# Loads of the values: window edges in two pieces, both batches in one request, values in fours split at partition 64

## The reference

```
# branch 1: positions averaged in fours (144 of them), full softmax attention, repeated 4 times
q_d = q.reshape(B, H, 144, 4, D).mean(axis=3)      # k_d, v_d likewise
out_up = np.repeat(softmax(q_d k_d^T / sqrt(D)) v_d, 4, axis=2)
# branch 2: every position attends to the positions less than 4 away
mask = np.abs(pos[:, None] - pos[None, :]) < 4
out_local = softmax(where(mask, q k^T / sqrt(D), -1e9)) v
x = (out_up + out_local) as 2304 tokens x 512
# layer 1: x / rms(x) * rms_g, then (silu(x w_gate) * (x w_val)) w_out, width 1536
# layer 2: relu(x w_in)^2 w_out, width 2048
```

## Time and profile before

| what | value |
|---|---|
| median of 3 runs | 960.91 us (960.46 to 963.03) |
| the profiled execution | 963.09 us |
| its span, first to last instruction | 961.3 us |
| mean granted TensorE clock | 0.978 |
| PE busy | 926.8 us, 96% |
| DVE, ACT, POOL busy | 648.3, 447.9, 588.7 us |
| DMA | 63.94 MB, mean 67 GB/s |

### The profile page before, as it was taken

The page is one execution under the profiler, slowest core; times in us unless marked ns, Lnnn a source line. Parts: engine busy times, 40 slices in busy tenths (PEclk is TensorE's granted clock), DMA queues, the critical chain, the costliest instruction groups (busy, mean ns, idle before and its releaser), DMA issues.

```text
span 961.3 us, 17765 instructions
## 1 busy us (share of the span) xinstructions
PE 926.8 (96%) x6056; PEld 837.6 (87%) x6056; DVE 648.3 (67%) x960; ACT 447.9 (47%) x1149; POOL 588.7 (61%) x627
## 2 busy tenths in 40 slices
PE   5879989999999999999999999999999999999998
PEld 5657768999999999999999998989898998989896
DVE  5859995678986668876455776667875456745353
ACT  3758785644455634455444464424342324333221
POOL 2458677778778867877766775555654445453520
PEclk9979878999999999999999999999999999999999
DMA  6566211321211111111111122121112101030101
GB/s 178 180 206 210 82 35 33 89 77 54 68 45 44 45 45 45 45 45 45 44 46 54 54 69 88 44 88 45 45 36 97 45 23 44 23 110 23 45 1 65
DMA packets 57961, 63.94 MB, mean 67 GB/s; under 512 B 5904, under 2 KB 50832, under 8 KB 57488
## 3 DMA queue, kind: packets, MB, share of 16 engines
q1 hardware_dynamic: 56288, 61.63, 20.8%
q10 hardware_dynamic: 1584, 1.18, 0.4%
HBM read 58.07 MB, written 4.72 MB: 65 GB/s over the span
## 4 chain that ended last, share of the span: by engine, by line
PE 77%; DVE 3%; issue 1%; ACT 1%; POOL 0%; DMA 0%; ACTq 0%; DVEq 0%
PE bank L1437 42%; PE bank L1492 20%; PE bank L1467 14%; DVE xs L1079 1%; ACT wst L698 0%; ACT xs L739 0%; DVE vt L1146 0%; DVE prod L1152 0%; PE bank L1447 0%; DVE wst L1086 0%; POOL wst L576 0%; DMA out_dram<-xT 0%; DVE gt L1146 0%; DVE wo L1191 0%; ACT xT L822 0%
## 5 line engine op out<-in xcount | busy, mean ns | idle before, releaser
L1437 PE MATMUL bank<-xs,wst 128*128 128x384 f32 x2520 | 505.1, 340 | 4.1 <-DVE vt L1146 2.4
L1437 PEld LDWEIGHTS bank<-xs,wst 128*128 128x128 f32 x2520 | 442.7, 189 | 28.6 <-issue 8.5
L576 POOL TENSOR_TENSOR wst<-wraw,wst 128x256 fp32r<-128x256 f32 x240 | 223.9, 952 | 143.0 <-ACT wst L698 141.7
L1492 PE MATMUL bank<-wo,gs 128*128 128x512 f32 x864 | 218.4, 393 | 1.4 <-ACT xT L822 0.8
L1467 PE MATMUL bank<-hb,wo 128*128 128x512 f32 x864 | 189.1, 336 | 1.3 <-DVE hb L1164 1.3
L1492 PEld LDWEIGHTS bank<-wo,gs 128*128 128x128 f32 x864 | 160.4, 188 | 29.8 <-DVE gs L1185 1.1
L1467 PEld LDWEIGHTS bank<-hb,wo 128*128 128x128 f32 x864 | 146.0, 188 | 9.9 <-issue 1.6
L1146 DVE TENSOR_TENSOR vt<-u,bank 128x384 f32<-128x384 f32 x120 | 66.2, 552 | 126.1 <-PE bank L1437 125.8
L698 ACT CAST wst<-wraw 128x256 fp32r<-128x256 f32 x360 | 123.1, 407 | 1.9 <-DMA wraw<-w_dram 1.2
L559 POOL TENSOR_TENSOR wraw<-wraw,stage 128x256 f32<-128x256 f32 x60 | 48.9, 815 | 96.5 <-DMA wraw<-w_dram 96.5
L785 ACT ACTIVATE sig<-gt 128x384 f32<-128x384 f32 x72 | 37.9, 526 | 124.8 <-DVE gt L1146 123.7
(11 more groups left out here) (110 smaller groups left out, 1054.5 us busy)
## 6 DMA issues: line engine op xcount, KB each, us to landing
wraw<-w_dram SPq DMA_DIRECT2D x180, 128.0 KB, 2.3
stage<-w_dram SPq DMA_DIRECT2D x60, 128.0 KB, 2.1
woraw<-w_dram SPq DMA_DIRECT2D x28, 256.0 KB, 3.0
vquad<-v_dram SPq DMA_DIRECT2D x16, 288.0 KB
out_dram<-xT SPq DMA_DIRECT2D x18, 256.0 KB, 2.9
vwin<-v_dram SPq DMA_DIRECT2D x56, 70.0 KB
kp<-k_dram SPq DMA_DIRECT2D x3, 1152.0 KB, 8.6
qs<-q_dram SPq DMA_DIRECT2D x3, 1152.0 KB, 11.0
```

Of the source, the lines that this page charges most:

```text
L576: nc.gpsimd.tensor_tensor(b[:, 1, :], w_source(w, p), b[:, 0, :].bitcast(fp32), ALU.subtract).then_inc(wlp_done, 1)
L1437: last = mm(XY[s % 2][:, 0:HC], wst[:, u % 2, p, pw, 128 * k:128 * k + 128], xs[:, p, px, k, :], start=(p not in CONTINUES and i == 0 and ...
L1492: last = mm(ACC[t][:, :], gs[:, v % 2, m, px, 128 * t:128 * t + 128], wo[:, 2 * j + m, pw, :], start=(j == 0 and n < 18 and i == 0), stop= ...
```

## The change

`load_v` now issues one request per unit for both batches of the group, with the batch as an inner dimension, where it issued two. For the first and the last unit, whose windows have 67 rows, it issues two such requests, of 64 and of 3 rows. That makes 11 requests per group where there were 18. `load_vquad` splits each of its four requests at partition 64, into 64 and 8 partitions. The waits count the new numbers of requests (`v_loads`, and 128 for 64 in `sum_values`). The same bytes go to the same places, in the same order on SyncE.

```diff
--- before.py
+++ after.py
@@ -389,6 +389,10 @@
         def head0(b):
             return NH * (b % 2)
 
+
+        def v_loads(u0, u1):
+            return u1 - u0 + (u0 == 0) + (u1 == NL)
+
         def down(g):
             i = g % NU - NL
             return i // 2, i % 2
@@ -405,21 +409,25 @@
         @block.sync
         def _(sp):
 
+
             def load_v(b, u0, u1, done):
                 for i in range(u0, u1):
                     t0, t1 = max(QB * i - HALO, 0), min(QB * i + QB + HALO, S)
-                    r0 = t0 - (QB * i - HALO)
-                    for x in range(2):
-                        src = v_d[batch0(b) + x][t0:t1, D * head0(b):D * head0(b) + GC]
-                        sp.dma_start(vwin[b % 2][r0:r0 + t1 - t0, x, i, :], src).then_inc(done, 16)
+                    r0 = QB * i - HALO
+                    for a, e in ((t0, t1),) if t1 - t0 == KW else ((t0, t0 + QB), (t0 + QB, t1)):
+                        src = v_d[batch0(b):batch0(b) + 2, a:e, D * head0(b):D * head0(b) + GC]
+                        sp.dma_start(vwin[b % 2][a - r0:e - r0, :, i, :],
+                                     src.rearrange("x r n -> r x n")).then_inc(done, 16)
+
 
             def load_vquad(b):
                 ready(sp, vd_done, 3 * b)
                 for x in range(2):
                     for kt in range(2):
                         v = v_d[batch0(b) + x][S // 2 * kt:S // 2 * kt + S // 2, D * head0(b):D * head0(b) + GC]
-                        sp.dma_start(vquad[:, kt, x, :, :],
-                                     v.rearrange("(p r) n -> p r n", r=FACTOR)).then_inc(vq_in, 16)
+                        fours = v.rearrange("(p r) n -> p r n", r=FACTOR)
+                        sp.dma_start(vquad[0:64, kt, x, :, :], fours[0:64]).then_inc(vq_in, 16)
+                        sp.dma_start(vquad[64:HK, kt, x, :, :], fours[64:HK]).then_inc(vq_in, 16)
 
             def rows_of(src, b, t0, t1):
                 return src[batch0(b):batch0(b) + 2, :, head0(b):head0(b) + NH, t0:t1].rearrange("b d h s -> (b d) h s")
@@ -980,7 +988,7 @@
             def sum_values(b, n):
 
                 if n == 0:
-                    dve.wait_ge(vq_in, 64 * (b + 1))
+                    dve.wait_ge(vq_in, 128 * (b + 1))
                     ready(dve, pv_done, NU * b)
                 else:
                     dve.wait_ge(vd_done, 3 * b + n)
@@ -1382,13 +1390,13 @@
                     pe.wait_ge(oe_done, g - 1)
                 if local(g):
                     if b == 0 and i == 0:
-                        pe.wait_ge(v_part[0], 32 * V_PARTS[0])
+                        pe.wait_ge(v_part[0], 16 * v_loads(0, V_PARTS[0]))
                     if b == 0 and i == V_PARTS[0]:
-                        pe.wait_ge(v_part[1], 32 * (V_PARTS[1] - V_PARTS[0]))
+                        pe.wait_ge(v_part[1], 16 * v_loads(V_PARTS[0], V_PARTS[1]))
                     if b == 0 and i == V_PARTS[1]:
-                        pe.wait_ge(v_in[b], 32 * (NL - V_PARTS[1]))
+                        pe.wait_ge(v_in[b], 16 * v_loads(V_PARTS[1], NL))
                     if b > 0 and i == 0:
-                        pe.wait_ge(v_in[b], 32 * NL)
+                        pe.wait_ge(v_in[b], 16 * v_loads(0, NL))
                     for x in range(2):
                         for a in range(NH):
                             c = QB * (2 * x + a // 2)
```

## The result

The changed kernel took 954.61 us as the median of 12 executions (947.97 to 961.93), the one before 960.94 (lowest 960.46). The ratio over all executions is 0.9921, interval 0.9892 to 0.9950, and that of the medians 0.9934: faster by 0.7 to 0.8%, where 1.6% was forecast, and just outside the range. But the profiled execution, the fastest of the twelve, took 947.97 us, 15.1 less than the profiled one before, and the forecast was 15.2. The median and the trace tell different stories because the executions of this kernel fall into two clusters. Of 24 timed (12 here, 12 in the run `again`) 9 lie from 947.9 to 953.1, 2 at 956 to 957, and 13 from 957.9 to 961.9. The mean clock goes with them: 0.983 to 0.989 in the first cluster, 0.971 to 0.978 in the last.

The account below looks back on a forecast made before the run. Bound: attention-stage loads on SyncE's queue, late because 67-row loads run on one engine. Gains 5.6 + 9.6 = 15.2 us took the profiled 963.09 to 947.9, median 945.7; forecast's own range 939 to 951, overall 939 to 954.

Parts of the forecast that it names:

- The mechanism of the gain: Attention stage: splitting 67-row loads takes away 11.4 us of one-engine work per group, so loads land before they are wanted.
- both waits: VectorE's 4.2 us wait for K's third piece and matmul's 7.6 us wait for group 1's windows, both forecast gone.
- the clock: Half-clock stretches from 100.3 and 131 us: may change, up to 4.7 us gained or 5 lost; taken as nothing.
- 5.6, 9.6 and 0: Forecast gains in us: up to Q of group 1, at group 1's windows, and from the late clock.
- Issue costs: SyncE's unblocked window requests per group: 7.2 us before, 5.6 after (4.1 to 9.2); group 1's issued by about 25 us.
- When the loads land: Attention stage: bytes set landing times at 278 GB/s after 5.6 us; K's third piece at 12.8 us, no wait left.
- Rival 3: Requests over two batches move slowly; at 70 GB/s group 1's windows land 19 us late: about 980 us; chance 0.03.
- Windows of group 1: They land at 32.7 us, wanted at 41.1; the 7.6 us matmul wait goes, gaining 9.6 us (7.6 to 10.4).
- one more stretch of 10 us: Rival 4: one more 10 us half-clock stretch in the part where matmul is full, 950.7 us; chance 0.05.
- Q of group 1 next late: Before unit 13: Q of group 1 lands at 28.1 us, wanted at 31.4; at 214 GB/s it lands at 34.8.
- rival 1: Loading group 1's K and Q replaces the wait: 949.2 us at 214 GB/s, 959.8 at 165, middle 954; chance 0.12.

Follow-up runs that it names:

- again: The changed kernel once more, unaltered; median 958.18 us (947.91 to 961.09), 12 executions, ratio to before 0.994.
- windows_only: The changed kernel with the `load_vquad` requests (the fours) left whole: merged windows with split edges; median 950.98 us, ratio to before 0.9887.
- edges_only: The kernel before with only the 67-row requests split into 64 and 3 rows, one request per batch, fours whole; median 949.85 us, ratio 0.9875.
- again_c: One more execution of the unaltered changed kernel, with its trace; 960.02 us.
- again_b: One more execution of the unaltered changed kernel, with its trace; 950.83 us.
- edges_gap: Kernel with only the 67-row requests split, where TensorE also waits before unit 8 for an otherwise unused 2 KB load; median 964.47 us, ratio to before 1.0018.

## Why the prediction was wrong

The mechanism of the gain was right. The 67-row loads on one engine were the cause of both waits, and their split is all of the gain. The step that failed is the clock: it was put at nothing, and in over half of the executions it takes back most of the gain. That the profile gave 15.1 us for a forecast of 15.2 is in part luck. It fell on the fastest execution, and its parts are 3.2, 9.9 and 2.0 us where 5.6, 9.6 and 0 were forecast. Against the steps:

- *Issue costs*: 5.95 us for the windows of group 0 (5.6 forecast). Those of group 1 took 10.99, single ones up to 2.60, and were handed over by 30.6 us, not 25. A pair of fours took 0.58 + 0.76 with the gaps (0.78 + 0.35). Their small half was the dearer one: 0.71 for eight partitions against 0.54 for 64, without the gaps.
- *When the loads land*: this step failed first in time. "With the work even over the engines, bytes set it", at 278 GB/s. Until 12 us the rate was as forecast, 286 GB/s, and the 2.93 MB up to K's third piece had been moved by about 12.5 us. But that piece landed at 14.9, not 12.8, when 3.27 MB had been moved; some of what was issued behind it had been moved before it was complete. So a wait of 1.38 us stayed. From 12 to 20 us the rate was 163. For Q of group 1 both add up: 7.18 MB were moved by about 30.5 us (28.1 forecast), and it landed at 33.66. Unit 13 began right behind it, 3.2 us earlier, not 5.6. Even work does not make the rate; the shape of what is mixed in the queues does. Rival 3 had merged requests as slow. By themselves they aren't (237 GB/s in windows_only, 227 in edges_only); with the split fours they are, in group 0.
- *Windows of group 1*: in time. The 9.6 us are 9.9 in the profile at 947.97 (13.1 less 3.2).
- *The clock*: this step put the result out of the range. I took nothing for it and gave 0.05 to one more stretch of 10 us. 13 of 24 executions are high; the one with a trace has 20.5 us at half clock, and it costs most of what the change gained: again_c is 9.2 us above again_b, of which 0.85 stand when the break ends and 8.0 more come in the half clock behind it. What is read as its cause, TensorE short of code behind the loads, was in none of the rivals. In the kernel before nothing of it showed: the packet landed at 17.5 us, and TensorE had done its 218th matmul at 24.6.
- *Q of group 1 next late* (rival 1): it lands at 33.7 where 28.1 was forecast. In the change the break hides it, since TensorE comes to unit 13 no sooner; in windows_only it is the 4.65 us.

The forecast of one number hid that the change moves the kernel next to two cliffs. Open are why merged windows and split fours together slow the packets, and why the clock stays at half for 20 us and more with TensorE busy; the first is shown by its parts, its mechanism isn't. That the break is a want of code is argued from times and counts, not shown by a run of its own.

## What to carry to other kernels

Look at how many rows a request has, not how many requests there are: 67 rows on one engine cost more than four extra requests. When loads are brought forward, look at what else comes through the DMA engines, the engines' own code too, and keep the queues from standing full where a code packet is due. Idle time of TensorE early in a light stage can cost more than its length, because the clock stays down after it: 7.28 us cost 14.8 in edges_gap. And time such a kernel many times, since one trace shows only one of its clusters. Try the parts of a change alone: here the edges by themselves are faster (949.85 us) than with the two parts that were added to them (954.61 and 958.18).

## What the runs showed of the hardware

- A matmul stream broke in the middle of a unit for 0.6 to 3.7 us, at a fixed place of the instruction stream, until 1.4 to 1.6 us after the end of a 16 KB code packet (seven traces).
- Loads that are issued later take part of the rate before an earlier one has landed: K's third piece landed when 3.27 MB had been moved, with 2.93 MB issued up to it.
- A 2 KB load, issued at 18.05 us into full queues, took 8.8 us to land.
- With all engines busy the same bytes moved at 163 or at 245 GB/s, by the shape of the requests alone: from 8.4 to 20 us its 1 KB packets took 101 ns on average in the one case, 73 in windows_only.
- Idle times of 3.2 to 3.7 us were followed by 20 to 27 us at half clock in three traces of the change and its kin; breaks of 0.6 to 1.6 us in four others were not. The idle time alone does not set the length: 10.2 us at half clock followed 7.6 us in the kernel before.
